# Softmax factor moved from the probabilities to the result of the value products

## The reference

```
q_bits = (q @ proj > 0); k_bits = (k @ proj > 0)      # 6 bits each, a bucket number
scores = where(same bucket, 0.125 * q @ k.T, -1e9)
p = exp(scores - max(scores)); p = p / (sum(p) + 1e-9)
x = (p @ v), heads side by side                        # 1536 tokens x 512
h = x @ w_in;  x = gate(h) @ w_out                     # 512 -> 2048 -> 512
h = x @ w_in2; out = (h - tanh(h)) @ w_out2
```

## Time and profile before

| | us |
|---|---|
| median of 3 runs (lowest, highest) | 793.65 (793.64, 794.2) |
| profiled execution | 793.87 |
| its span | 792.0 |
| busy in the span: PE, DVE, ACT, POOL | 767.6, 423.0, 356.5, 327.2 |
| granted clock, mean | 0.994 |

### The profile page before, as it was taken

How to read it: one execution, slowest core, us unless ns; L and a number is a source line. 1 busy time by engine, 2 the same in 40 slices (tenths; PEclk the granted TensorE clock), 3 DMA queues, 4 the chain that set the end, 5 groups by cost and what they waited for, 6 DMA issues and landing times.

```text
span 792.0 us, 11765 instructions
## 1 busy us (share of the span) xinstructions
PE 767.6 (97%) x3712; PEld 638.6 (81%) x3712; DVE 423.0 (53%) x757; ACT 356.5 (45%) x701; POOL 327.2 (41%) x267
## 2 busy tenths in 40 slices
PE   4999999999999999999999999999999999999998
PEld 2888888888888888878887888878888888888886
DVE  2899999999997665443334455551223221231213
ACT  2889888889885333342333323331212221221212
POOL 4789889889899994000000276760000000000000
PEclk8899999999999999999999999999999999999999
DMA  6633523423232342000000023220001000010001
GB/s 191 171 114 105 160 75 114 151 80 115 67 106 63 124 134 81 0 1 1 0 1 0 26 80 106 80 80 1 0 1 52 2 0 0 0 53 0 0 0 53
DMA packets 17864, 47.25 MB, mean 60 GB/s; under 512 B 2288, under 2 KB 4464, under 8 KB 17840
## 3 DMA queue, kind: packets, MB, share of 16 engines
q1 hardware_dynamic: 17840, 46.94, 18.8%
HBM read 38.87 MB, written 3.15 MB: 53 GB/s over the span
## 4 chain that ended last, share of the span: by engine, by line
PE 81%; POOL 5%; issue 4%; DVE 3%; ACT 3%; DMA 2%; SPq 1%; DVEq 0%; POOLq 0%; ACTq 0%
PE ps L497 34%; PE ps L574 30%; PE ps L474 5%; PE ps L488 5%; PE ps L460 3%; PE ps L463 3%; PE ps L431 2%; POOL probs L354 2%; POOL k_b L339 1%; ACT probs L619 1%; DMA k_raw<-kk 1%; DVE g_raw L813 1%; ACT g_hi L701 1%; DVE row_den L743 1%; POOL q_b L311 1%
## 5 line engine op out<-in xcount | busy, mean ns | idle before, releaser
L497 PE MATMUL ps<-x_hi,w 128*128 (+1 forms) x768 | 255.2, 397 | 0.0
L821 DVE TENSOR_TENSOR g_lo<-g_raw,g_hi 128x512 fp32r<-128x512 f32 x96 | 72.9, 759 | 269.1 <-ACT g_hi L701 269.1
L701 ACT ACTIVATE g_hi<-g_raw 128x512 fp32r<-128x512 f32 x96 | 60.7, 632 | 296.2 <-PE ps L574 270.2
L497 PEld LDWEIGHTS ps<-x_hi,w 128*128 128x128 f32 x768 | 144.5, 188 | 33.8
L497 PE MATMUL ps<-x_lo,w 128*128 (+1 forms) x384 | 152.2, 396 | 0.0
L574 PE MATMUL ps<-g_hi,w 128*128 128x512 f32 x384 | 125.6, 391 | 2.5 <-DVE g_lo L821 2.5
L574 PE MATMUL ps<-w,g_hi 128*128 128x512 f32 x384 | 118.7, 390 | 0.0
L311 POOL TENSOR_SCALAR w<-stage 128x1024 fp32r<-128x1024 f32 x32 | 38.8, 1212 | 164.5 <-PE ps L574 161.9
L751 DVE TENSOR_TENSOR p_lo<-ps,p_hi 128x384 fp32r<-128x384 f32 x192 | 98.0, 552 | 9.3 <-ACT p_hi L629 7.5
L354 POOL TENSOR_SCALAR probs<-probs,row_inv 128x768 f32<-128x768 f32 x96 | 86.9, 910 | 23.9 <-DVE row_inv L745 23.0
L629 ACT ACTIVATE p_hi<-ps 128x384 fp32r<-128x384 f32 x192 | 84.9, 489 | 24.5 <-PE ps L474 22.3
(11 more groups left out here) (48 smaller groups left out, 905.2 us busy)
## 6 DMA issues: line engine op xcount, KB each, us to landing
stage<-weights SPq DMA_DIRECT2D x32, 512.0 KB, 3.3
qk_raw<-qk SPq DMA_DIRECT2D x16, 384.0 KB, 3.5
q_raw<-qq SPq DMA_DIRECT2D x16, 384.0 KB, 3.2
k_raw<-kk SPq DMA_DIRECT2D x16, 384.0 KB, 3.8
q_a<-q_b SPq DMA_DIRECT2D x16, 192.0 KB
v_raw<-v SPq DMA_DIRECT2D x16, 192.0 KB, 2.6
out<-stage SPq DMA_DIRECT2D x12, 256.0 KB, 2.1
q_b<-bits SPq DMA_DIRECT2D x16, 54.0 KB
```

The source lines that it names most:

```text
L497: last = nc.tensor.matmul(ps[:, f % H_BANKS, :], w[:, f, wp, k * P:(k + 1) * P], xs[:, k, bass.ds(t * TOK, TOK)], start=(k == 0 and wp == ...
L701: nc.scalar.activation(g_hi[:, slot, :], g_raw[:, slot, :], ACT.Copy).then_inc(g_hi_ready, 1)
L821: nc.vector.tensor_tensor(g_lo[:, slot, :], g_raw[:, slot, :], g_hi[:, slot, :].bitcast(F32), ALU.subtract).then_inc(g_split, 1)
```

## The change

The probabilities are transposed unscaled, straight after the exponent. The factors of a head (768) are written by one DMA to DRAM and read back by another, spread over the 64 partitions that hold the head's result; POOL then multiplies `x_pair` by them, once a pair. `x_hi` and `x_lo` come from the scaled `x_pair`. The lags are 3 (transposes, p_hi, p_lo), 7 (value products) and 9 (low half, fold) instead of 5, 9 and 11; the scaling stands at POOL's turn 9 - 3 = 6, `x_lo` and `x_hi` of the old pair at turn 7. POOL rounds k in place of ACT. The inverse is taken once for six tiles, at turns 1 and 7. For pair 7, DVE scales and splits x by halves, in the drain. The second early weight chunk is split at turn 8.

```diff
-SCALE_LAG = 3
-TRANSPOSE_LAG = 5
-PV_LAG = 9
-FOLD_LAG = 11
+TRANSPOSE_LAG = 3
+PV_LAG = 7
+FOLD_LAG = 9
+SCALE_TURN = FOLD_LAG - HT
...
+            x_tiles = x_pair[:, :].rearrange("p (o q) -> p o q", o=QT)
+            inv_tiles = inv_wide[:, :].rearrange("p (q o) -> p o q", o=QT)
...
+            def store_inv(p, s):
+                sp.wait_ge(inv_ready, 2 * p + s + 1)
+                sp.dma_start(factors[2 * p + s, :].rearrange("(q o) -> q o", o=QT), row_inv[:, s, :])\
+                    .then_inc(inv_stored[s], 16)
+
+            def spread_inv(p, s):
+                sp.wait_ge(inv_stored[s], 16 * (p + 1))
+                if s == 0:
+                    wait_from(sp, x_scaled, p)
+                sp.dma_start(inv_wide[s * D:(s + 1) * D, :], factors[bass.ds(2 * p + s, 1), :].broadcast_to([D, S]))\
+                    .then_inc(inv_spread, 16)
...
             def pair(p):                              # SP
+                if not first:
+                    store_inv(p - 1, 1)
                 sp.wait_ge(qk_split, 2 * p + 2)
                 copy_q_hi(1)
                 copy_bits(1)
+                if not first:
+                    spread_inv(p - 1, 1)
...
                 sp.wait_ge(qk_split, 2 * p + 3)
                 copy_q_hi(0)
                 copy_bits(0)
+                store_inv(p, 0)
                 if not before:
                     load_qk(2 * p + 4, 0)
+                spread_inv(p, 0)
...
             load_w(0, 0)
             load_w(1, 1)
+            for s in range(2):
+                store_inv(PAIRS - 1, s)
+                spread_inv(PAIRS - 1, s)
...
             def split_k(p, s):                        # POOL
+                pool_round(k_a[:, s, :], k_raw[:, s, :]).then_inc(k_hi_ready, 1)
                 pool.wait_ge(k_hi_ready, 2 * p + s + 1)
...
-            def normalise(p, o):
-                wait_alone(pool, inv_ready, 4 * p + o // HT + 1, pool_passed)
-                pool.tensor_scalar(probs[:, o % QT, :], probs[:, o % QT, :], row_inv[:, o % QT:o % QT + 1], 1.0,
-                                   ALU.mult, ALU.mult).then_inc(probs_ready, 1)
+            def scale_x(p):
+                wait_alone(pool, folded, 4 * (p + 1), pool_passed)
+                wait_alone(pool, inv_spread, 32 * (p + 1), pool_passed)
+                pool.tensor_tensor(x_tiles, x_tiles, inv_tiles, ALU.mult).then_inc(x_scaled, 1)
...
                 for n in range(PT_TILES):             # POOL
-                    old = trailing(p, n, SCALE_LAG)
-                    if old and not (drain and n >= SCALE_LAG):
-                        normalise(*old)
+                    old = trailing(p, 0, 1)
+                    if old and n == SCALE_TURN and not drain:
+                        scale_x(old[0])
+                    if old and n == SCALE_TURN + 1 and not drain:
+                        split_x(old[0])
...                                                  # then split_q at 0 and 6, split_k at 1 and 7
-                        if last and n in (5, 7):
-                            split_w((n - 5) // 2)
-                    if n == 9 and not drain:
-                        old = trailing(p, 0, 1)
-                        if old:
-                            split_x(old[0])
+                        if last and n in (5, 8):
+                            split_w((n - 5) // 3)
...
             def transposes(p, o):                     # PE
-                pe.wait_ge(probs_ready, PT_TILES * p + o + 1)
+                pe.wait_ge(exp_done, PT_TILES * p + o + 1)
...
             def round_x(p):                           # ACT
-                act.wait_ge(folded, 4 * (p + 1))
+                act.wait_ge(x_scaled, p + 1)
...
                 for n in range(PT_TILES):             # ACT, in this order
                     parts_hi of tile n - 3
+                    if old and old[1] % HT == 0: lower_half (tile n - 9)
+                    if old and n == SCALE_TURN + 1 and not drain:
+                        round_x(old[0])
                     if not drain:
-                        if n == 0:
-                            round_k(p, 1, PT_TILES * p)
-                        if n == 6 and not (isinstance(p, int) and p == PAIRS - 1):
-                            round_k(p + 1, 0, PT_TILES * p + QT)
                         exponent(p, n)
...
-            def invert(p, k):                         # DVE, at every third turn
+            def invert(p, s):                         # DVE, at turns 1 and 7
+                dve.wait_ge(exp_done, PT_TILES * p + QT * (s + 1))
...
                 for n in range(PT_TILES):             # DVE, in this order
                     clamp(p, n); parts_lo of tile n - 3
+                    if old and old[1] % HT == 0: fold (tile n - 9)
+                    if drain and n in (SCALE_TURN - HT, SCALE_TURN):
+                        scale_last_x(n // SCALE_TURN)
+                    if drain and n in (SCALE_TURN - HT + 1, SCALE_TURN + 1):
+                        split_last_x((n - SCALE_TURN - 1) // HT + 1)
+                    if n % QT == 1: invert the six tiles before
```

More of the change, by code:

```diff
@@ L85, in trailing, with build @@
     return None if isinstance(p, int) and p < 0 else (p, o)
-def build(nc, qq, kk, qk, v, mask_consts, weights, out):
+def build(nc, qq, kk, qk, v, mask_consts, weights, factors, out):
     ctx = ExitStack()
@@ L127, in build @@
             row_min = sb("row_min", [P, QT], F32, att)
-            row_sum = sb("row_sum", [P, QT], F32, att)
-            row_den = sb("row_den", [P, QT], F32, att)
-            row_inv = sb("row_inv", [P, QT], F32, att)
+            row_sum = sb("row_sum", [P, 2, QT], F32, att)
+            row_den = sb("row_den", [P, 2, QT], F32, att)
+            row_inv = sb("row_inv", [P, 2, QT], F32, att)
+            inv_wide = sb("inv_wide", [P, S], F32, att)
+            x_tiles = x_pair[:, :].rearrange("p (o q) -> p o q", o=QT)
+            inv_tiles = inv_wide[:, :].rearrange("p (q o) -> p o q", o=QT)
         w = sb("w", [P, FC, 2, CH], F32R)
@@ L171, in build @@
         inv_ready = sem("inv_ready")
-        probs_ready = sem("probs_ready")
+        inv_stored = [sem(f"inv_stored{s}") for s in range(2)]
+        inv_spread = sem("inv_spread")
+        x_scaled = sem("x_scaled")
+        x_last_scaled = sem("x_last_scaled")
         part_ready = sem("part_ready")
@@ L263, in pair @@
                 before = isinstance(p, int) and p == PAIRS - 2
+                first = isinstance(p, int) and p == 0
+                if not first:
+                    store_inv(p - 1, 1)
                 sp.wait_ge(qk_split, 2 * p + 2)
@@ L278, in pair @@
                 copy_bits(0)
+                store_inv(p, 0)
                 if not before:
                     load_qk(2 * p + 4, 0)
+                spread_inv(p, 0)
                 sp.wait_ge(v_split, 2 * p + 2)
                 load_v(2 * p + 3, 1)
-            with sp.Fori(0, PAIRS - 2) as p:
+            pair(0)
+            with sp.Fori(1, PAIRS - 2) as p:
                 pair(p)
@@ L410, in _ @@
             pair(PAIRS - 1)
-            pair(PAIRS, drain=True)
             pool.wait_ge(scores_ready, PAIRS * PT_TILES)
@@ L620, in exponent @@
                                      bias=row_min[:, n % QT:n % QT + 1], scale=-1.0,
-                                     accum_out=row_sum[:, n % QT:n % QT + 1]).then_inc(exp_done, 1)
+                                     accum_out=row_sum[:, n // QT, n % QT:n % QT + 1]).then_inc(exp_done, 1)
             def parts_hi(p, o):
@@ L636, in lower_half, with round_k @@
                 nc.scalar.activation(low[:, k % 2, :], ps[D:P, PV0 + k % 2, 0:HALF], ACT.Copy).then_inc(low_ready, 1)
-            def round_k(p, s, tiles_before):
+            def round_k(p, s):
                 act.wait_ge(qk_loaded[s], 32 * (p + 1))
-                wait_from(act, scores_ready, tiles_before)
                 nc.scalar.activation(k_a[:, s, :], k_raw[:, s, :], ACT.Copy).then_inc(k_hi_ready, 1)
             def round_x(p):
-                act.wait_ge(folded, 4 * (p + 1))
+                act.wait_ge(x_scaled, p + 1)
                 nc.scalar.activation(x_hi_flat[:, bass.ds(rows(p), S)], x_pair[:, :], ACT.Copy)\
@@ L648, in round_last_x @@
             def round_last_x(half):
-                act.wait_ge(folded, 4 * PAIRS - 1 + half)
+                act.wait_ge(x_last_scaled, half + 1)
                 cols = slice(rows(PAIRS - 1) + half * HALF, rows(PAIRS - 1) + (half + 1) * HALF)
@@ L656, in pair @@
                 for n in range(PT_TILES):
[L657 to L665, removed]
                     old = trailing(p, n, TRANSPOSE_LAG)
@@ L668, in pair @@
                         parts_hi(*old)
+                    old = trailing(p, n, FOLD_LAG)
+                    if old and old[1] % HT == 0 and not (drain and n >= FOLD_LAG):
+                        lower_half(old[0], old[1] // HT)
+                    old = trailing(p, 0, 1)
+                    if old and n == SCALE_TURN + 1 and not drain:
```

(37 more changed lines are left out.)

## The result

The changed kernel takes 824.44 us (median of 4 runs, 822.15 to 826.41) where the kernel before takes 793.64; the ratio is 1.0384 [1.0368, 1.0401]. The profiled execution took 824.08 with a span of 822.1. Forecast were 808 and a range of 802 to 822: the sign and the place were right, the size was not. The time went up 30.2 us, not 14.5.

What follows compares the result with a forecast made beforehand. PE with small waits bounds the attention stage. Pair 1 at 42.0, six pairs of 31.25 (187.5), pair 7 26.8 and 25.3 after give 281.6 instead of 267.1: 793.65 + 14.5 = 808, range 802 to 822.

Steps and rivals of the forecast that it cites:

- The chain: Before pairs 2 to 7: fold, scaling x, five POOL passes, row copies; next scores 17.6 us after tile 6's, PE waits 3.4.
- The size of scaling x: POOL's scaling pass, once a pair: 1.83 us taken, upper end 2.58, reading factors 24 bytes apart.
- The half pair without a chain: Tile 0 to tile 6 of a pair: no such chain, 13.7 us with one bit product and 0.2 of local waits.
- The clock: Rival: PE's wait brings the clock to half; 833 in all six pairs, 816 to 830 in a few; chance 0.12.
- The tail: From pair 7's start to the second matrix's first products: 26.8 us for pair 7, then 25.3.
- the wait for weights: After pair 7, weights 2 and on load behind the last inverse's store and spread; with other waits PE waits 4.6 us.
- a wrong term: Pair 7, before 28.4 us: without bit products and k to split 24.7, plus about 2 for ACT's wait, 26.8.
- the drain: From pair 7's end to the second matrix's first products: PE work 20.7 us plus waits 4.6, 25.3.
- The sum: Whole kernel: second matrix starts at 281.6 instead of 267.1, so +14.5 us, 808 us.
- the start -1.5: Pair 0: longer lags add two tiles' transposes and value products, 2.6 us; pair 1 starts near 42.0 instead of 39.66.
- the slow read: Rival: strided read makes scaling x 2.6 to 2.7 us, chain 0.8 longer before six pairs, 813; chance 0.18.
- The gain that was looked for: Attention pairs: POOL nets -6.9 us a pair, ACT -1.5, all off PE; a wait returns at most 1.7 a pair.

Runs made afterwards that it cites:

- number 1: Against the changed kernel, the scaling of x moved behind the split of k in POOL's order, same turn 6; 800.59 us, 1.0082 of the kernel before.
- number 3: Against the changed kernel, scaling reads the spread factors in the order in which they lie, so they meet the wrong columns; 820.7 us, 1.0365 of the kernel before.
- number 11: Scaling behind split of k, weights 2 and 3 ahead of last factors, x rounded and split at turn 8, threshold ahead of inverse's sum, against changed kernel; 790.03 us.
- number 4: Against the changed kernel, PE does 24 transposes of the identity at the end of pairs 1 to 6, inside the wait for row copies; 819.29 us, 1.0322.
- numbers 1 and 2: The second of these: against the changed kernel, only the split of x moved behind the split of k, scaling stays ahead; 817.8 us, 1.0297.
- number 8: Against the changed kernel, scaling behind split of k, weights 2 and 3 ahead of last factors, x rounded and split at turn 8; 794.08 us, 1.0004.
- number 7: Against the changed kernel, scaling behind the split of k, and weights 2 and 3 loaded ahead of the last head's factors; 797.19 us, 1.0044.

## Why the prediction failed, by its steps

*The chain.* Each link held: fold at T+3.8 (T+3.7 forecast), scaling at T+4.7 (4.5: it starts 0.34 after its releaser, not 0.19), five passes behind it, copies 3.9, no gap anywhere. Undoing the order alone gave back 24 us, the clock's part among them, as the wait went. Shown by number 1.

*The size of scaling x.* 2.23 us, between the ends of 1.83 and 2.58; I took the lower. With the 0.2 before it this puts tile 0 at T+18.1 instead of 17.6. Shown by number 3: unstrided it is 1.83. The Trainium skill, GPSIMD Engine Reference, section on performance pitfalls for Q7 kernels, has half as much again per element for such a step; here the row is 22% longer, and the measurement decides.

*The half pair without a chain.* 14.2 us, not 13.7 (106.27 to 120.51). The excess stands at turns 2 and 3, which take 2.2 and 2.5 us instead of 2.06. With ACT's wait for scaled x gone and the sum of turn 1 not held up (number 11) the half still takes 14.06, and a whole pair 28.7, 1.4 above PE's own 27.3. What that rest is was not tried.

*The clock: the step that failed.* I had one fall in the trace of before, 4.1 us after PE stopped, and took the wait of 3.4 as safe, with 0.12 for the rival. The table has PE's wait before a pair (before pair 7 some differ, 1.2 to 3.9) and how many of the six pairs 2 to 7 had a stretch at half clock at their start. It is from one execution of each kernel, and the counts can differ in others: the changed kernel's four runs have mean granted clocks of 0.979 to 0.988, the longest time with the lowest.

| kernel | wait, us | of 6 |
|---|---|---|
| changed | 3.1 | 5 |
| plain read | 3.1 | 3 |
| k rounded by ACT | 2.2 | 4 |
| split of x behind k | 1.9 | 3 |
| old lags | 1.6 to 1.9 | 2 |
| PE kept at work | 0.5 | 0 |
| scaling behind k | up to 0.5 | 0 |

It fell after waits well below 4.1 us, not each time, and sometimes a while after PE had resumed (with the split of x behind k PE resumed at 104.5 and the clock fell at 106.4). In the pairs of the changed kernel each low stretch lasted 3.4 us and cost 1.2 to 1.4: tile 0 to tile 6 takes 14.2 us without one and 15.4 to 15.6 with, not the 4 to 5 more that I took from the 10 us at the start. So the rival's condition was too strict and its price three times too high. Four of the five falls lie in the pairs 1 to 6 and cost 5.0 us by these rows, 4.2 by number 4; the fifth, in pair 7, cost 1.3. That the wait brings the clock down rests on numbers 1 and 4, the last two rows of the table. Why it fell after some waits and not after others of the same length stays open.

*The tail.* 57.5 us, not 52.1. I had the wait for weights at the right place. Its rows, POOL, then PE, of the changed kernel, from the start of pair 7 to the second matrix:

```profile
281.56 1.35 POOL L342 TENSOR_SCALAR w<-stage 128x1024 fp32r<-128x1024 f32 x1 [12.32 <-DMA stage<-weights]
283.00 2.81 POOL L401 TENSOR_TENSOR w<-stage,w 128x1024 fp32r<-128x1024 f32 x1
```

```profile
239.86 0.59 PE L489 MATMUL ps<-k_a,q_a 128*128 128x384 f32 x2 [3.61 <-issue]
...
285.86 0.79 PE L526 MATMUL ps<-x_hi,w 128*128 128x512 f32 x1 [3.18 <-POOL w L401]
...
294.41 0.50 PE L526 MATMUL ps<-x_hi,w 128*128 128x512 f32 x1 [1.32 <-POOL w L401]
...
297.32 0.39 PE L603 MATMUL ps<-g_hi,w 128*128 128x512 f32 x1
```

The weights were asked for at 276.73, landed 4.8 us later (3.3 forecast) and took 4.2 to split; PE waited 3.2 and 1.3, near the 4.6 of the forecast. Of the 5.4 us too few, 2.4 lie in pair 7, which took 29.2 us up to its last value products instead of 26.8: 1.3 for the fall of the clock at 241.1 (number 1, without one, takes 28.0), 1.2 for a wrong term. I took bit products out of pair 7, but it had none before the change either, and took 28.4 all the same. The rest lies in the drain, 28.2 instead of 25.3. The fall of the clock there (at 285.5) is not the reason: without one, numbers 1 and 2 take 28.0 and 28.3, as PE then comes earlier to weights that are not ready. In number 1, PE waits 5.7 of these 28.0 and works 22.3, against 4.6 and 20.7 in the forecast. What the 1.6 us of work are was not followed.

*The sum.* The missing is 30.2 - 14.5 = 15.7 us. The six pairs of 33.2 instead of 31.25 are 11.9 of it: 3.4 the chain (0.57 each), 3.0 the other half (0.5 each), 5.0 the clock, 0.5 a longer second half of pair 6, which I can't name. The tail is 5.4, the start -1.5. I had set the slow read and the clock as rivals, each with its own time; they came together with the forecast, and their sum lies above the range. The clock's 6.3 us (5.0 and 1.3) decide it: without them the time would be about 818 by this estimate, inside the range, and number 4 measured 819.3.

*The gain that was looked for.* POOL's 57 us and ACT's 7 bought nothing as long as the order was wrong, and little after: 790.03 against 793.91 of the kernel before, measured beside it, a ratio of 0.9944 [0.9922, 0.9965]. How much of this comes from moving the factor is not shown. Part of it is the luck of turn 1, and the kernel before was never run with x split later or with the threshold ahead of the sum, though its own sum is held up too (last section).

## What to carry to other kernels

An engine that works in a written order is late by what stands at the head of its queue, not by how busy it is: before a step is moved, list what it waits for, what is queued behind it, and who waits for that. When a repair gives less than its wait was long, compare the pair half by half: a second wait may stand beside the first, or a new one far from it. And one clock fall in a trace shows that a wait can bring the clock down, not how long a wait is safe.

## What the runs showed of the hardware

A small DVE instruction is held up by a POOL instruction that started before it, one with two inputs or with one (number 8, turn 1). `row_den`, 128x6 elements, takes 0.16 us when POOL is idle, and also when POOL's instruction starts 0.02 us after it (106.63 and 106.65 in number 7). In the changed kernel at turn 7 it takes 0.76 and ends at 127.48, as scaling x does (125.21 + 2.23). Begun 2.0 instead of 1.5 us into POOL's pass, it shrinks to 0.26 and ends with it again. DVE and POOL rows, first of the changed kernel, then of the one with the threshold ahead:

```profile
126.72 0.76 DVE L765 TENSOR_SCALAR row_den<-row_sum 128x6 f32<-128x6 f32 x1
```

```profile
119.34 2.24 POOL L391 TENSOR_TENSOR x_pair<-x_pair,inv_wide 128x768 f32<-128x768 f32 x1 [1.36 <-DVE x_pair L788]
...
121.34 0.26 DVE L768 TENSOR_SCALAR row_den<-row_sum 128x6 f32<-128x6 f32 x1
```

I had read the long rows of this sum in the kernel before as a wait for the exponent. Its own trace has it otherwise, DVE then POOL:

```profile
128.75 1.01 DVE L743 TENSOR_SCALAR row_den<-row_sum 128x3 f32<-128x3 f32 x1
```

```profile
128.72 1.02 POOL L348 TENSOR_TENSOR v_s<-v_raw,v_s 128x384 fp32r<-128x384 f32 x1
```

Both end at 129.75. The Trainium skill, SBUF — State Buffer, section "Who interferes with whom", says that VectorE's `tensor_scalar` can run in a two-port mode, and that then it and a GpSimd instruction lock each other out, whichever starts first keeping the other waiting to its end: by that rule, the trace agrees, to 0.04 us. That this sum ran in such a mode no trace here shows.
